# A fused attention and two-layer MLP kernel: a new order of work at the passage from attention to the MLP

## The reference

```python
scores = q @ k.T / sqrt(D) + min(-(cum_i - cum_j), 0), causal   # cum = cumsum(relu(s))
attn   = softmax(scores) @ v                        # (4, 8, 576, 64)
x      = attn.transpose(0, 2, 1, 3).reshape(2304, 512)
h      = x @ w_in                                   # (2304, 1024)
solu   = h * softmax(h)
ln     = (solu - mean) / sqrt(var + 1e-6) * g_ln
x2     = ln @ w_out                                 # (2304, 512)
out    = maximum(x2 @ w1, x2 @ w2, x2 @ w3) @ w_out2
```

## Time and profile before

| what | value |
|---|---|
| median of 3 runs | 754.85 us (753.32 to 757.14) |
| profiled execution, its own time | 754.38 us |
| its span | 752.6 us, mean granted TensorE clock 0.993 |
| PE busy | 712.0 us (95%) |
| PEld busy | 661.7 us (88%) |
| DVE, ACT, POOL busy | 399.4 us (53%), 319.1 us (42%), 255.0 us (34%) |
| DMA | 59.47 MB, mean 79 GB/s |
| chain that ended last | PE 74%, DVE 8%, issue 4%, ACT 4%, DMA 4%, SP's queue 3%, POOL 2% |

### The profile page before, as it was taken

One profiled execution on the slowest core, in us unless ns is written; L12 is line 12 of the kernel. 1 busy time (PEld: TensorE's weight loads), 2 busy tenths in 40 slices (PEclk: granted clock), 3 DMA queues, 4 the chain that ended last, 5 costly groups with the idle time before them and its releaser, 6 DMA issues.

```text
span 752.6 us, 12597 instructions
## 1 busy us (share of the span) xinstructions
PE 712.0 (95%) x4248; PEld 661.7 (88%) x4248; DVE 399.4 (53%) x702; ACT 319.1 (42%) x763; POOL 255.0 (34%) x284
## 2 busy tenths in 40 slices
PE   2889999999889799999999999999999999999998
PEld 2788888888778599989898999989989999899996
DVE  8889999999856755544445365503213123032120
ACT  1788888898764243333323244312112121121111
POOL 6857679898768743707010100000000000000000
PEclk9999999999999999999999999999999999999999
DMA  7689988889675303540000031000010000100101
GB/s 162 134 196 208 201 188 193 187 192 209 148 172 116 85 14 71 119 134 1 1 0 1 1 112 57 1 28 15 1 43 1 15 28 1 42 0 0 42 0 42
DMA packets 58230, 59.47 MB, mean 79 GB/s; under 512 B 23572, under 2 KB 45204, under 8 KB 58164
## 3 DMA queue, kind: packets, MB, share of 16 engines
q1 hardware_dynamic: 58196, 59.02, 33.4%
HBM read 44.15 MB, written 10.10 MB: 72 GB/s over the span
## 4 chain that ended last, share of the span: by engine, by line
PE 74%; DVE 8%; issue 4%; ACT 4%; DMA 4%; SPq 3%; POOL 2%; DVEq 0%; ACTq 0%; POOLq 0%
PE ps L674 10%; PE ps L675 10%; PE ps L673 10%; PE ps L591 4%; PE ps L592 4%; PE ps L593 4%; PE ps L518 4%; PE ps L519 4%; PE ps L520 4%; PE ps L690 3%; PE ps L689 3%; PE ps L688 3%; PE ps L484 3%; DVE nmax L1083 2%; PE ps L606 2%
## 5 line engine op out<-in xcount | busy, mean ns | idle before, releaser
L675 PE MATMUL ps<-x_lo,w_hi 128*128 (+1 forms) x432 | 144.4, 334 | 0.0
L673 PE MATMUL ps<-x_hi,w_hi 128*128 128x384 f32 x432 | 144.3, 334 | 0.0
L674 PE MATMUL ps<-x_hi,w_lo 128*128 128x384 f32 x432 | 144.3, 334 | 0.0
L868 ACT ACTIVATE probs<-ps,nmax 128x576 f32<-128x576 f32 (+4 forms) x160 | 82.9, 538 | 14.4 <-DVE nmax L1083 14.4
L1090 DVE TENSOR_TENSOR pt_lo<-ps,pt_hi 128x512 fp32r<-128x512 f32 (+1 forms) x128 | 78.2, 652 | 13.7 <-ACT pt_hi L878 10.5
L484 PE MATMUL ps<-ident,probs 128*128 128x128 f32 x480 | 76.2, 284 | 9.2 <-DVE pt_lo L1090 6.3
L466 PE MATMUL ps<-k_a,q_a 128*128 128x288 f32 (+2 forms) x192 | 63.2, 337 | 19.4 <-DVE q_a L1076 12.8
L674 PEld LDWEIGHTS ps<-x_hi,w_lo 128*128 128x128 f32 x432 | 81.1, 188 | 0.2
L673 PEld LDWEIGHTS ps<-x_hi,w_hi 128*128 128x128 f32 x432 | 81.1, 188 | 0.2
L675 PEld LDWEIGHTS ps<-x_lo,w_hi 128*128 128x128 f32 x432 | 81.1, 188 | 0.0
L878 ACT ACTIVATE pt_hi<-ps 128x512 fp32r<-128x512 f32 (+1 forms) x128 | 69.7, 573 | 18.0 <-PE ps L484 16.0
(11 more groups left out here) (100 smaller groups left out, 1454.1 us busy)
## 6 DMA issues: line engine op xcount, KB each, us to landing
qk_raw<-in_qk_dram SPq DMA_DIRECT2D x64, 288.0 KB, 4.6
xT<-halves SPq DMA_DIRECT2D x32, 144.0 KB, 2.7
xb_dram<-halves SPq DMA_DIRECT2D x32, 144.0 KB, 2.5
xb<-xb_dram SPq DMA_DIRECT2D x24, 192.0 KB, 3.7
rinvB<-rsum_dram SPq DMA_DIRECT2D x24, 192.0 KB, 4.4
stage<-in_moe_w_dram SPq DMA_DIRECT2D x18, 256.0 KB, 4.6
out_dram<-stage SPq DMA_DIRECT2D x18, 256.0 KB, 2.0
v_raw<-in_v_dram SPq DMA_DIRECT2D x32, 128.0 KB, 4.2
```

What stands on the lines that cost most here:

```text
L673: pe.matmul(dst, w_hi[f][:, i, c, :], x2_hi[par][:, c, :], start=(c == 0), stop=False)
L674: pe.matmul(dst, w_lo[f][:, i, c, :], x2_hi[par][:, c, :], start=False, stop=False)
L675: mm = pe.matmul(dst, w_hi[f][:, i, c, :], x2_lo[:, c, bass.ds(g * GT, GT)], start=False, stop=(c == KC - 1))
L868: act.activation(dst, SCORES[c], ACT.Exp, bias=nmax[par][:, c:c + 1], accum_out=sums_all[:, c, bass.ds(t, 1)]).then_inc(exp_done, 1)
```

## The change

The changed kernel has the same instructions but for two: at the start two negated copies go from DVE to ACT (L1069 and L1071 before). The rest is order.

- Start: POOL clears `qk_b` first and its other constants after; DVE's four small memsets of `q_a` and `qk_b` come behind `cum_lo`; ACT makes `ncum_hi` and `ncum_lo`, and SP waits for both (`cum_ready >= 2`).
- SP: `load_xb(1)` stands ahead of `load_rinv(1)`.
- POOL: slot 32 (the low piece of v of head 31) ahead of `join(1)`; `join(2)` right behind the high pieces of w_out, so ahead of `normalize(0, 0)`; each high piece of w_out has its own increment of `wout_hi_ready`.
- ACT and DVE: the split of x tile (0, 0) stands between slots 31 and 32, so behind ACT's copy of halves and ahead of the first `pt_high` and `pt_low` of slot 32; that of tile (0, 1) takes its old place within slot 32.
- PE: in slot 32 `values(PV_A)` comes ahead of the first half of `hidden(0, 0)`.
- DVE in group 0: `wout_low` as 3 pieces behind tile 0, one within tile 1, one within tile 2 (between the row maximum and the wait for the exponential), 3 behind tile 2. `invert_sums(2)` moves from behind tile (0, 0) to behind tile (1, 0).

```diff
@@ sync
-            sp.wait_ge(cum_ready, 1)
+            sp.wait_ge(cum_ready, 2)
...
             store_x(HEADS - 4, 0)
+            load_xb(1)
             load_rinv(1)
-            load_xb(1)
@@ tensor, slot
-                if known == HEADS:
-                    pe.wait_ge(win_hi_ready, WPIECES)
-                    pe.wait_ge(win_lo_ready, WPIECES)
-                    hidden(0, 0, 0, (0,))
...
                     values(t, par, 6, PV_A)
+                if known == HEADS:
+                    pe.wait_ge(win_hi_ready, WPIECES)
+                    pe.wait_ge(win_lo_ready, WPIECES)
+                    hidden(0, 0, 0, (0,))
...
-            pe.wait_ge(wout_hi_ready, 1)
+            pe.wait_ge(wout_hi_ready, FB)
@@ gpsimd
+            for i in range(2):
+                pool.memset(f32(qk_b[i][:, PAD:SP + S]), 0.0).then_inc(rows_zeroed, 1)
             for m in (ident, ident_b, mask):
...
             slot(HEADS - 1, 1, HEADS - 1)
+            slot(HEADS, 0, HEADS)
             join(1)
-            slot(HEADS, 0, HEADS)
             divide(1, 1)
...
             for f in range(FB):
-                hi = pool.tensor_scalar(wout_hi[:, f, :], ...)
-            hi.then_inc(wout_hi_ready, 1)
+                pool.tensor_scalar(wout_hi[:, f, :], ...).then_inc(wout_hi_ready, 1)
+            join(2)
...
-                    if i == 0 and more and ahead:
+                    if i == 0 and more and ahead and not first:
                         join(g + 2)
@@ scalar
+            act.wait_ge(cum_step, 4)
+            act.activation(ncum_hi, cum_hi, ACT.Copy, scale=-1.0).then_inc(cum_ready, 1)
+            act.wait_ge(cum_step, 5)
+            act.activation(ncum_lo, cum_lo, ACT.Copy, scale=-1.0).then_inc(cum_ready, 1)
...
                 if known == HEADS:
-                    act.wait_ge(q_lo_ready, HEADS)
-                    act.wait_ge(k_lo_ready, HEADS)
-                    x_high(0, 0, 0, True)
+                    x_high(0, 1, 1, True)
...
+            act.wait_ge(q_lo_ready, HEADS)
+            act.wait_ge(k_lo_ready, HEADS)
+            x_high(0, 0, 0, True)
             slot(HEADS, 0, HEADS)
-            x_high(0, 1, 1, True)
@@ vector
-            dve.tensor_scalar(ncum_hi, cum_hi, -1.0, None, ALU.mult)
-            dve.wait_ge(cum_step, 5)
-            dve.tensor_scalar(ncum_lo, cum_lo, -1.0, None, ALU.mult).then_inc(cum_ready, 1)
...
                 if known == HEADS:
-                    x_low(0, 0, 0)
+                    x_low(0, 1, 1)
...
-            for t in range(HEADS - 4, HEADS + 1):
+            for t in range(HEADS - 4, HEADS):
                 slot(t, t % 2, t)
-            x_low(0, 1, 1)
+            x_low(0, 0, 0)
+            slot(HEADS, 0, HEADS)
...
-                dve.wait_ge(wout_hi_ready, 1)
                 for f in fs:
+                    dve.wait_ge(wout_hi_ready, f + 1)
...
                 dve.tensor_reduce(st[:, 0:1], h, AX_X, ALU.max, negate=True).then_inc(hmax_done, 1)
+                if first and i > 0:
+                    wout_low(range(i + 2, i + 3))
                 dve.wait_ge(e_done, t + 1)
...
                     if first and i == 0:
-                        invert_sums(2)
-                    if first and i == 1:
                         wout_low(range(0, 3))
                     if first and i == 2:
-                        wout_low(range(3, FB))
+                        wout_low(range(5, FB))
+                    if last_sums and i == 0:
+                        invert_sums(2)
...
-            group(1, 1, False)
+            group(1, 1, False, last_sums=True)
```

18 lines of the change are left out of this document (8 added, 10 removed).

## The result

| | before | changed kernel |
|---|---|---|
| median, first comparison | 756.0 us (753.32 to 757.74, 4 runs) | 745.75 us (745.12 to 748.0, 4 runs) |
| ratio to before, 95% interval | | 0.9886 (0.9853 to 0.9918) |
| once more, beside the last experiments | 756.04 us (17 runs) | 746.87 us (746.14 to 748.67, 6 runs), 0.988 (0.9852 to 0.9907) |
| span of the profiled run | 752.6 us | 743.3 us |
| granted TensorE clock, mean | 0.993 | 0.997 |

The kernel is 1.1% faster. The prediction, 749.3 us, was on the right side and its range held the time; it gave 3.55 us too little.

A forecast was written before the change was run, and what follows sets the result against it. PE, busy 95% of the span, bounds the kernel, with waits to win ahead of its steady part. 9.0 (passage) + 1.1 (start) - 3.8 (new wait) - 1.2 (clock) = 5.1 us off 754.38: 749.3 us, range 744.0 to 753.0.

The forecast's parts named there:

- First split and first half of hidden: At the first hidden: x_lo ready earlier, hidden starts 1.9 us sooner, at full clock, six products no longer behind; 4.1 us won.
- Tile (0, 1): DVE before this tile's maximum: three low pieces of w_out replace the inversion, 3.15 us against 2.0; 1.1 us lost.
- The dear rate: Tile (0, 1): low pieces at the full price of the dearer row, slowed beside POOL; 2.1 us lost, sum 1.0 smaller.
- Tile (0, 2) and the turn: Group 0: 3.41 us wait goes, 3.4 won; turn's wait 2.07 falls to 1.2, 0.9 won; clock stays up, 1.7 won.
- Passage: From the last head into group 0: terms 4.1 - 1.1 + 3.4 + 0.9 + 1.7, sum 9.0 us won.
- The inversion, moved: Group 1: xb(3)'s load queues behind the inversion in SP, delaying POOL's join(3) and normalisations; new PE wait 3.8 us at turn_ln(1).
- The clock behind it: Half clock on PE after the new wait at turn_ln(1): between nothing and 1.7 us, taken as 1.2 us lost.
- Start: Kernel's start: shorter DVE chain, earlier q_low(0), reload(2, 0) then held by POOL's low piece of k; 1.1 us won, bounds 0.2 to 1.4.
- against 1: Rival: no new wait at turn_ln(1), stores land faster or PE's chain is later; 10.1 us won, 744.3 us; chance 0.12.
- against 2: Rival: DVE stays late in group 0, low pieces 1.36 us each, half clock as before; 753.0 us, no change; chance 0.17.
- against 3: Rival: late xb loads don't catch up, turn_ln waits in groups 1, 2 and 3; 760.8 us, slower; chance 0.05.
- against 4: Rival: only the start moves or fails; within the forecast's own range, given no separate chance.

The follow-up runs named there:

- the last version above: Changed kernel with SP loading xb(3) ahead of its wait for the inverted sums, and the aux-row store moved behind reload(2): 742.12 us, ratio 0.9819.
- xb(3) freed: Changed kernel with SP issuing the load of xb(3) ahead of its wait for the inverted sums: 742.38 us, ratio 0.9815.
- the passage alone: Kernel before with all of the change except the start edits, so low pieces of w_out and inversion as changed: 752.97 us, ratio 0.998.
- the start alone: Kernel before with only the start edits (qk_b cleared first, negated copies on ACT, DVE's small memsets later): 750.4 us, ratio 0.9923.
- its three parts: Kernel before with one start edit each: negated copies on ACT, 753.93 us; POOL clearing qk_b first, 752.31 us; DVE's pad memsets later, 757.12 us.
- the store behind the reload: Kernel before with SP's 576 KB store of aux rows moved behind reload(2): 753.84 us, ratio 0.9972.
- the inversion put back: Changed kernel with the inversion back behind tile (0, 0), ahead of the three low pieces: 745.89 us, ratio 0.9866.

## Why the prediction was right, and where it was short

- *First split and first half of hidden.* Foreseen: 4.1. PE begins the first product of hidden 5.44 us behind the last head's first exponential (214.13 less 208.69) where it was 7.24: 1.8, of 1.9 predicted, and at full clock. Undone by itself it costs 4.7, with a wait 0.7 longer than that of before. Right.
- *Tile (0, 1).* 1.1 lost was predicted, at 1.05 for a piece. The three took 2.94, 0.98 each, and the wait grew from 0.37 to 1.26: 0.9 lost. In the last version above (xb(3) freed, store behind the reload) they took 2.42, and the wait was 0.46. The dear rate of 2.1 lost, which the prediction set beside the Trainium skill's "GPSIMD Engine Reference", section Key points, did not come.
- *Tile (0, 2) and the turn.* The wait of 3.41 went whole, as predicted. The turn kept 0.62 us, not 1.2: POOL's last normalisation took 1.77 us beside DVE's three pieces where I let it end a single microsecond sooner than 2.94. The clock stayed up: 12 transposes in 1.50, front to back 4.10. Passage: 9.0 predicted, 9.9 measured.
- *The inversion, moved.* The wait came where, by whom and for the reason that the prediction gave: 4.11 us of 3.8. With xb(3) freed it was gone.
- *The clock behind it.* 1.2 predicted, 1.7 measured (2.3 with the passage alone). What was mis-sized here is "nothing as after 3.41, where the first product took 0.47". A first product of 0.47 doesn't show that the wait was free. In the start alone PE's first product behind 2.57 us takes 0.47 too, and half clock sets in 1.0 us later, in the fifth product; the 12 products take 4.36 us (218.29 to 222.65) against 2.7:

```profile
218.29 0.47 PE L518 MATMUL ps<-win_hi,x_hi 128*128 128x512 f32 x1 [2.57 <-DVE x_lo L1115]
...
219.06 0.39 PE L518 MATMUL ps<-win_hi,x_hi 128*128 128x512 f32 x1
219.29 0.58 PE L519 MATMUL ps<-win_lo,x_hi 128*128 128x512 f32 x1
219.66 0.63 PE L520 MATMUL ps<-win_hi,x_lo 128*128 128x512 f32 x1
```

- And the row behind the 3.41 us was the exception. In before the clock stays at 1.00 up to the next wait, 3.0 us later. In the five other traces with this code (the start alone, its three parts, the store behind the reload) the first product behind the same wait (3.40 to 3.43) takes 0.76 or 0.77, the clock is 0.50, the way to the turn takes 5.25 us and not 3.00, and the turn has no wait left. From the start alone:

```profile
251.00 0.76 PE L518 MATMUL ps<-win_hi,x_hi 128*128 128x512 f32 x1 [3.41 <-DVE x_lo L1115]
...
256.25 1.78 PE L606 MATMUL ps<-ident,ln 128*128 128x128 f32 x12
```

- So the 2.07 us and the half clock behind them, 2.6 of the sum of 9.0, are costs of this one trace; elsewhere the half clock stood in their place, 1.1 us cheaper together, which is most of what the tail of before is longer than the others. From the last head's first exponential to S the five take 51.0 to 52.2 us. By the Trainium skill's "TensorE: Matmul & The Clock Gate", section What's actually happening, as weighed in the prediction, the term would have been the full 1.7, and the row of the new wait bears it out.
- *Start.* 1.1 predicted with bounds 0.2 to 1.4; 2.7 to 3.1 at the heads 0 to 4, and 5.2 in the traces at the last head. **This is the step that failed**, in two places. "POOL's cleared rows change place at no cost" gave them nothing, but in the trace of before they held DVE's relu at 1.72 us; I had looked at what the memsets cost POOL, and not at who stood beside them. And "then waits for POOL's low piece of k, which ends at 11.14: 1.3 us at most" took POOL's first pieces as they were, 0.92 and 1.16 us, though DVE's cast, subtraction and first negated copy (6.63 to 9.05) lay beside them; now DVE is through with these before POOL begins, and they take 0.67 and 0.66, and the low piece ends at 10.58. The rest of the 2.7 is the load's landing, 5.8 us from issue to POOL's copy in place of 6.7, with the aux store 2.0 and not 1.0 us ahead.
- *From head 4 to head 31.* The rest of the gain, 2.5 us, was not predicted, and only in part does it go with the change. This stretch took 172.79 us in the trace of before and 170.33 after, but 171.76 in the second trace of the changed kernel and 172.79 with the start alone. All 14 traces run from 170.33 to 178.45. From head 4 to head 27 the traces with the whole changed start took 142.5 to 144.3 us but for one (149.3, the inversion put back), those without it or with a part of it 144.7 to 147.6. Most of that difference stands in one step, from head 4 to head 5: 6.17 to 6.62 us with the whole changed start (9.68 in the one exception), 7.33 to 8.52 without it, 7.83 in before. This and the medians of the start alone, 5 us, speak for a gain here; why the start should shorten that step stays open, as no run was made on it.

That the tail's 4.1 us agree so well with the 4.0 is partly luck: the passage gave 0.9 more than its terms, and the new wait and its clock took 0.8 more (4.11 and 1.67 against 3.8 and 1.2), and against the mean of the other traces it is 3.1. What came out right by its mechanism is the three waits that went, the one that came, and its cause.

Of the rivals, none came: PE waited at the turn of group 1 (against 1), DVE was in time with pieces of 0.98 (against 2), group 2 had no wait (against 3), and the passage paid (against 4).
